# Transposes of p ahead of a unit's first tile, banks that change places in odd units, and the product by q first on VectorE

## The reference

```python
# 1: a linear attention with complex decays; B, H, S, D = 4, 8, 768, 48
mag = np.sqrt(a_re * a_re + a_im * a_im)
scale = np.minimum(mag, 0.999) / (mag + 1e-06)
for t in range(S):
    new_re = ar * S_re - ai * S_im          # a * scale, at t
    new_im = ar * S_im + ai * S_re
    S_re, S_im = new_re + kv, new_im        # kv: outer product of k and v at t
    y[:, :, t] = np.einsum('bhd,bhde->bhe', q[:, :, t], S_re)
# 2: a feed-forward layer, 384 -> 2048 -> 384, on N = 3072 tokens
h = x @ w_in
g = np.where(h >= 1, h, np.where(h <= -1, 0.0, (h + 1) ** 2 / 4.0))
x = g @ w_out
# 3: eight experts, 384 -> 1024 -> 384, weighted by a normalized gate
P = np.exp(x @ w_gate - max);  8 times: rows, then columns of P normalized
out = sum over e of P[:, e:e + 1] * (np.maximum(x @ w1[e], 0.0) @ w2[e])
```

## Time and profile before

| | |
|---|---|
| median of 3 runs | 2386.37 us (2386.13 to 2387.14) |
| the profiled execution | 2386.86 us, span 2385.1 us |
| TensorE, matmuls | 2261.7 us, 95% of the span |
| VectorE | 1559.6 us, 65% |
| ScalarE | 981.6 us, 41% |
| GpSimd | 461.0 us, 19% |
| mean granted TensorE clock | 0.989 of 2.4 GHz |

### The profile page before, as it was taken

How to read it: one execution, slowest core, us unless ns; L and a number is a source line. 1 busy time by engine, 2 the same in 40 slices (tenths; PEclk the granted TensorE clock), 3 DMA queues, 4 the chain that set the end, 5 groups by cost and what they waited for, 6 DMA issues and landing times.

```text
span 2385.1 us, 43991 instructions
## 1 busy us (share of the span) xinstructions
PE 2261.7 (95%) x16891; PEld 2241.0 (94%) x16891; DVE 1559.6 (65%) x2953; ACT 981.6 (41%) x1675; POOL 461.0 (19%) x325
## 2 busy tenths in 40 slices
PE   2689999999999989999999999999999999999999
PEld 2689999999999889999999999999999999999999
DVE  6898888888874685555556666555556655565553
ACT  2455555555555433333333433333333333333331
POOL 0000000000000312222222222122222222222221
PEclk9799999999999999999999999999999999999999
DMA  3211111111112310011112211110013211111101
GB/s 105 84 33 48 49 49 49 49 50 49 50 37 71 120 54 24 31 54 54 55 54 93 94 54 54 55 53 25 32 54 117 70 54 54 54 54 54 54 1 27
DMA packets 73194, 132.46 MB, mean 56 GB/s; under 512 B 5608, under 2 KB 36584, under 8 KB 72936
## 3 DMA queue, kind: packets, MB, share of 16 engines
q1 hardware_dynamic: 72936, 129.14, 16.4%
HBM read 114.96 MB, written 14.16 MB: 54 GB/s over the span
## 4 chain that ended last, share of the span: by engine, by line
PE 81%; DVE 10%; ACT 7%; issue 2%; DMA 0%; DVEq 0%; ACTq 0%; SPq 0%
PE bank L1431 13%; PE bank L1433 13%; PE bank L1432 13%; PE bank L1598 11%; PE bank L1599 11%; PE bank L1600 11%; PE bank L1412 2%; PE bank L1418 2%; PE bank L1417 2%; PE bank L1422 1%; ACT ubuf L648 1%; ACT ubuf L650 1%; PE bank L1407 1%; ACT ubuf L646 1%; DVE tmp L861 1%
## 5 line engine op out<-in xcount | busy, mean ns | idle before, releaser
L1431 PE MATMUL bank<-x_h,w_h 128*128 128x256 f32 x2112 | 595.8, 282 | 9.0 <-issue 4.1
L1433 PE MATMUL bank<-x_h,w_l 128*128 128x256 f32 x2112 | 595.0, 282 | 0.0
L1432 PE MATMUL bank<-x_l,w_h 128*128 128x256 f32 x2112 | 594.1, 281 | 0.0
L1598 PE MATMUL bank<-w_h,h_h 128*128 128x384 f32 x1536 | 518.2, 337 | 0.4 <-DVE acc L1233 0.4
L1600 PE MATMUL bank<-w_h,h_l 128*128 128x384 f32 x1536 | 515.0, 335 | 0.0
L1599 PE MATMUL bank<-w_l,h_h 128*128 128x384 f32 x1536 | 514.9, 335 | 0.0
L567 POOL TENSOR_TENSOR h_l<-u_s,h_h 128x512 fp32r<-128x512 f32 x192 | 244.6, 1295 | 1136.6 <-ACT h_h L778 1136.6
L1431 PEld LDWEIGHTS bank<-x_h,w_h 128*128 128x128 f32 x2112 | 400.7, 190 | 11.9 <-issue 6.0
L1432 PEld LDWEIGHTS bank<-x_l,w_h 128*128 128x128 f32 x2112 | 401.9, 190 | 0.0
L1433 PEld LDWEIGHTS bank<-x_h,w_l 128*128 128x128 f32 x2112 | 401.5, 190 | 0.0
L1240 DVE SCALAR_TENSOR_TENSOR acc<-bank,prob,acc 128x384 f32<-128x384 f32 x168 | 103.5, 616 | 370.6 <-PE bank L1600 370.6
(11 more groups left out here) (164 smaller groups left out, 4035.8 us busy)
## 6 DMA issues: line engine op xcount, KB each, us to landing
stage<-w_ SPq DMA_DIRECT2D x48, 768.0 KB, 7.9
w_raw<-w_ SPq DMA_DIRECT2D x96, 384.0 KB, 4.8
qb<-q_in_ SPq DMA_DIRECT2D x24, 192.0 KB
kb<-k_in_ SPq DMA_DIRECT2D x24, 192.0 KB
vb<-v_in_ SPq DMA_DIRECT2D x24, 192.0 KB
x_hi<-x2h_s SPq DMA_DIRECT2D x36, 128.0 KB, 1.8
x_lo<-x2l_s SPq DMA_DIRECT2D x36, 128.0 KB, 1.8
x_h<-x_hi SPq DMA_DIRECT2D x6, 768.0 KB, 4.4
```

The costliest lines, as they stand in the source:

```text
L1431: pe.matmul(dst, w[0], x[0], start=first, stop=False)
L1432: pe.matmul(dst, w[0], x[1], start=False, stop=False)
L1433: return pe.matmul(dst, w[1], x[0], start=False, stop=last)
L1598: pe.matmul(dst, h_h[:, f, t_], w2s[slot][0][:, f], start=n == 0, stop=False)
```

## The change

On TensorE steps 0 and 1 stand before the first mm_in of a unit instead of behind it. They wait for p and for state_add of the unit before; for the rest of the unit before step 2 waits. So that this can be, step_bank(u, i) uses the three banks in the order 0, 1, 2 in even units and 0, 2, 1 in odd ones, and step 12 uses the bank of step 10. The gate's matmuls move between steps 0 and 1, ahead of mm_in, and write into columns that step 1 leaves alone.

On VectorE the product by q is the first of the unit, ahead of gate_out and g_lo(t-1). p_inv of an even unit moves from the end of the odd unit before into the even unit, behind g_lo(t-1). final moves ahead of state_add at an odd unit's end. scale(u + 3) moves ahead of g_max(t+3) and x_lo.

On ScalarE, in even units: p_sq behind g_hi(t), stacks(u, 1) ahead of p_root, scale_sq(u + 3) ahead of g_sq(t+2), scale_root(u + 3) ahead of g_hi(t+2).

```diff
+        def step_bank(u, i):
+            return att[(i if u % 2 == 0 else -i) % 3] if i < 12 else step_bank(u, 10)
...
@@ ScalarE, unit(u) @@
                 stacks(u, 0)
-                if even:
+                if even and not moe:
                     p_sq(u + 1)
...
                 if u > 2:
                     g_hi(t)
+                if even and moe:
+                    p_sq(u + 1)
                 if moe:
                     g_sq(t + 1)
+                stacks(u, 1)
                 if even:
                     p_root(u + 1)
-                stacks(u, 1)
                 if moe:
                     g_hi(t + 1)
-                    g_sq(t + 2)
                 if even and u + 3 < UNITS:
                     scale_sq(u + 3)
+                if moe:
+                    g_sq(t + 2)
...
+                if even and u + 3 < UNITS:
+                    scale_root(u + 3)
                 if moe:
                     g_hi(t + 2)
                     g_sq(t + 3)
-                if even and u + 3 < UNITS:
-                    scale_root(u + 3)
...
@@ VectorE, unit(u) @@
+                by_qk(u, 0)
+                if not even and u >= 5:
+                    gate_out(u // 2 - 2)
+                if u == 1:
+                    scale(3)
                 if u > 2:
                     g_lo(t - 1)
-                if not even and u >= 5:
-                    gate_out(u // 2 - 2)
-                by_qk(u, 0)
-                if u == 1:
-                    scale(3)
+                if even:
+                    p_inv(u)
                 if u > 2:
                     g_max(t)
...
                 if scans:
                     scan(pair, 1, 4)
+                    final(u + 1)
                 state_add(u)
...
-                if scans:
-                    final(u + 1)
+                if even and u + 3 < UNITS:
+                    scale(u + 3)
                 if moe:
                     g_max(t + 3)
...
                 x_lo(u)
-                if even and u + 3 < UNITS:
-                    scale(u + 3)
-                if scans:
-                    if u + 3 < UNITS:
-                        scale_sum(u + 3)
-                    p_inv(u + 1)
+                if scans and u + 3 < UNITS:
+                    scale_sum(u + 3)
...
@@ TensorE @@
                 if i == 0:
                     pe.wait_ge(p_done, u + 1)
-                    if u:
-                        pe.wait_ge(dve_ev, d)
-                        pe.wait_ge(act_ev, a)
-
+                if i == 1 and u:
+                    pe.wait_ge(dve_ev, (u - 1) * DVE_EV + 7)
+                    if u % 2 and u >= 5:
+                        gate(u // 2 - 2)
                 if i == 2:
+                    pe.wait_ge(act_ev, a)
                     pe.wait_ge(dve_ev, d + 2)
...
-            STEPS_AT = [(), (0, 1), (2, 3), (4, 5), (6, 7), (8, 9), (10, 11), (12,)]
+            STEPS_AT = [(0, 1), (), (2, 3), (4, 5), (6, 7), (8, 9), (10, 11), (12,)]
```

More of the change, by code:

```diff
@@ L627, in stacks @@
                     act.activation((qs, ks)[half][0:96, 4 * n:4 * n + 4],
-                                   att[i % 3][0:96, :].rearrange("p (h t) -> p h t", h=4), ACT.Copy)\
+                                   step_bank(u, i)[0:96, :].rearrange("p (h t) -> p h t", h=4), ACT.Copy)\
                        .then_inc(act_ev, 1)
@@ L632, in y_out @@
                 act.wait_ge(step_done, u * STEPS + (12 if u < 2 else 11))
-                act.activation(y, att[1][:, 0:DM], ACT.Copy).then_inc(act_ev, 1)
+                act.activation(y, step_bank(u, 10)[:, 0:DM], ACT.Copy).then_inc(act_ev, 1)
             def x_hi(u):
@@ L637, in x_hi @@
                 act.activation(xh[:, u // 2 % 2, :, of_unit(u, 128)],
-                               att[0][:, 0:DM].rearrange("p (k t) -> p k t", k=KT), ACT.Copy).then_inc(act_ev, 1)
+                               step_bank(u, 12)[:, 0:DM].rearrange("p (k t) -> p k t", k=KT), ACT.Copy)\
+                   .then_inc(act_ev, 1)
             def g_sq(t):
@@ L961, in bound @@
                 dve.wait_ge(step_done, u * STEPS + 6)
-                dve.tensor_reduce(r_sum[0:1, u:u + 1], att[2][0:1, DM:DM + KT + 1], AX.X, ALU.add).then_inc(bound_done, 1)
+                dve.tensor_reduce(r_sum[0:1, u:u + 1], step_bank(u, 5)[0:1, DM:DM + KT + 1], AX.X, ALU.add)\
+                   .then_inc(bound_done, 1)
             def by_qk(u, half):
@@ L978, in masked @@
                     dve.wait_ge(step_done, u * STEPS + 9 + n)
-                    dve.tensor_tensor(at[:, 4 * n:4 * n + 4], att[(8 + n) % 3][:].rearrange("p (h t) -> p h t", h=4),
-                                      mask[:].unsqueeze(1).to_broadcast([128, 4, 128]), ALU.mult).then_inc(dve_ev, 1)
+                    dve.tensor_tensor(at[:, 4 * n:4 * n + 4],
+                                      step_bank(u, 8 + n)[:].rearrange("p (h t) -> p h t", h=4), mask[:].unsqueeze(1).to_broadcast([128, 4, 128]), ALU.mult).then_inc(dve_ev, 1)
             def state_add(u):
@@ L984, in state_add @@
                 dve.wait_ge(step_done, u * STEPS + 12)
-                dve.tensor_tensor(state[0:96, b, 0:DM], att[2][0:96, 0:DM], state[0:96, b, 0:DM], ALU.add).then_inc(dve_ev, 1)
+                dve.tensor_tensor(state[0:96, b, 0:DM], step_bank(u, 11)[0:96, 0:DM], state[0:96, b, 0:DM], ALU.add)\
+                   .then_inc(dve_ev, 1)
             def x_lo(u):
@@ L1362, in att_step @@
                 d, a = u * DVE_EV, u * ACT_EV
-                dst = att[i % 3]
+                dst = step_bank(u, i)
                 if i == 0:
                     pe.wait_ge(p_done, u + 1)
-                    if u:
-                        pe.wait_ge(dve_ev, d)
-                        pe.wait_ge(act_ev, a)
+                if i == 1 and u:
+                    pe.wait_ge(dve_ev, (u - 1) * DVE_EV + 7)
+                    if u % 2 and u >= 5:
+                        gate(u // 2 - 2)
                 if i == 2:
+                    pe.wait_ge(act_ev, a)
                     pe.wait_ge(dve_ev, d + 2)
+                if i == 4:
+                    pe.wait_ge(pinv_done, u + 1)
                     if u % 2 and u >= 5:
                         pe.wait_ge(lg_done, u // 2 - 1)
-                if i == 4:
-                    pe.wait_ge(pinv_done, u + 1)
                 if i == 5:
@@ L1470, in gate @@
                     tok = slice(b * 128, (b + 1) * 128)
-                    o = b * 2 * E
+                    o = DM + b * 2 * E
                     for n in range(KT):
@@ L1489, in _ @@
                         mm_in(t)
-                    if s == 0 and u % 2 and u >= 5:
-                        pe.wait_ge(dve_ev, (u - 1) * DVE_EV + 7)
-                        gate(u // 2 - 2)
                     for i in STEPS_AT[2 * s + 1]:
```

6 lines of the change are left out of this document (3 added, 3 removed).

## The result

The changed kernel takes 2406.64 us (median of four runs, 2402.94 to 2407.74), the kernel before, run beside it, 2386.25 us (four runs, 2384.96 to 2387.14). The ratio is 1.0083, with an interval from 1.0066 to 1.0101: the change makes the kernel 20 us slower. The forecast was 2412 us.

A forecast was written before the change was run, and what follows sets the result against it. TensorE, busy 95% of the span, was taken to bound the kernel, so its work and gaps count. 2386.9 + 15 (waits in nine pairs) + 10 (clock) + 0 (other units) = 2412 us; 8 in 10 range 2391 to 2425.

The forecast's parts named there:

- What the change removes: TensorE's gaps per pair of units: on qt 1.31 and 0.95, on ks 0.95; together 3.2 us removed.
- Step 1, pinv: Even unit: p_inv behind the product by q and g_lo makes TensorE wait 0.8 us for pinv (0 to 1.5).
- Step 2, kt: Even unit: final's first instruction, held beside GpSimd's pinv, delays the product by k; new TensorE wait 1.35 us.
- Step 3, at: Even unit: masked ends at 291.17, TensorE would be there at 291.06; new wait 0.1 us (0 to 0.9).
- Step 4, x2l_s: Even unit: squaring waits for the decays' reload, g_sq through x2_lo queue behind; first mm_out waits 2.6 us (0.9 to 3.5).
- Step 5, the odd unit: Odd unit: product by q comes without a gap, kt and at just in time; 0.05 us added; pair 61.0.
- The other units: Units 1, 2, 22 and 23, outside the nine full pairs: together 0 us, from -4 to +2.
- The clock: TensorE's clock halves for 3.4 us after the 2.6 us gap in two of three pairs, 1.7 us each: +10 us.
- Slower, but at full clock: Rival, chance 0.31: the waits as forecast but no clock drop; 2402 us, from 2393 to 2407.
- Faster: Rival, chance 0.13: reload no obstacle, x2_lo done by 298.5, 2.6 us sooner; 2378 us, at best 2352.
- It evens out: Rival, chance 0.06: hold shorter than in unit 2 (-1.05) and x2_lo 1 us earlier; 2387 us.
- worse: Rival, chance 0.05: the odd unit's thin margins go too, by a us each; over 2425 us.

The follow-up runs named there:

- steps_back: Changed kernel with squaring behind third g_sq, p_inv ahead of g_lo, and TensorE's steps 0 and 1 behind mm_in again: 2360.3 us; in five rounds 2359.0.
- old_banks: Kernel before, its banks and TensorE order kept, with the change's ScalarE and VectorE order except squaring behind g_sq, p_inv ahead of g_lo: 2363.17 us.
- pinv_first: Changed kernel with p_inv of even units moved ahead of g_lo(t - 1) on VectorE: 2399.64 us, ratio 1.0052.
- x2_first: Changed kernel with scale_sum(u + 3) of even units moved behind x2_lo on VectorE: 2399.76 us, ratio 1.0055.
- sq_back: Changed kernel with scale_sq(u + 3) put back behind g_sq(t + 2) on ScalarE: 2373.23 us, ratio 0.9940.
- two_bufs: Changed kernel with a second buffer for the decays of odd units from unit 5 on, loaded one release earlier: 2374.26 us, ratio 0.9953.
- sq_ahead: Kernel before with only scale_sq(u + 3) moved ahead of g_sq(t + 2) in even units: 2395.89 us, ratio 1.0038.
- ks_first: Kernel before with only stacks(u, 1) moved ahead of p_root on ScalarE: 2381.06 us, ratio 0.9979.
- order_only: Kernel before with stacks(u, 1) ahead of p_root, VectorE's product by q first and even units' p_inv ahead of g_lo: 2382.17 us, ratio 0.9988.

## Why the prediction was right

**What the change removes.** Right: neither qt nor ks is waited for in the steady part, 3.2 us per pair. But the text put the qt gaps down to the early transposes and the order on VectorE together. steps_back and old_banks show that in the steady part the order does it alone.

**Step 1, pinv.** 0.8 forecast, 0.80 in unit 8 (0.74 to 0.91 in nine units). pinv_first removed it by the edit that the step implies.

**Step 2, kt.** 1.35 forecast, 1.31 measured. The hold of final's first instruction by pinv was 1.06 us (1.61 against 0.55), forecast 1.05 from the row of unit 2. A row from another place of the program, of the same two instructions, was a good price. The Trainium skill, "SBUF — State Buffer", section "SBUF: two separate sides", says that a VectorE instruction with two inputs in SBUF and a GpSimd instruction that reads SBUF share a port pair as an exclusive lock, which the one that starts first holds for its whole length. The traces agree: 1.61, 2.20 and 2.19 us beside pinv, and 0.75 in x2_first, where scale_sum came 0.3 us before pinv's end. There state_add and x2_lo, which read one input from a bank, stand beside the same pinv (299.22, 1.83 us) and aren't held:

```profile
299.25 0.55 DVE L994 TENSOR_TENSOR state<-bank,state 96x384 f32<-96x384 f32 x1
299.72 1.07 DVE L1015 TENSOR_TENSOR x2l_s<-bank,x2h_s 128x256 fp32r<-128x256 f32 x3
300.71 0.75 DVE L841 SCALAR_TENSOR_TENSOR sqa<-sqa 128x384 f32<-128x384 f32 x1
```

**Step 3, at.** 0.1 forecast, 0.16 to 0.22 measured.

**Step 4, x2l_s.** ScalarE's wait near 5 forecast and 4.87 measured; VectorE's some 4 and 3.92; the mm_out's 2.6 and 2.1 to 2.3, two of 2.72 and 2.83 behind late reloads (mean of the nine 2.3). The chain of single-buffer reload, squares, g_max, p_inv, scale_sum, x2_lo stood as walked. sq_back and two_bufs, which cut it at two different places, gave back 33 and 32 us, and sq_ahead put it into the kernel before for 9. What the sum could not say, and x2_first did, is that the last link is exchangeable: with scale_sum out of the way the pair is 0.1 us shorter, no more, at full clock.

**Step 5, the odd unit.** No gap, as forecast. The pair came out at 60.97 us against 61.0. That it agrees so closely is in part luck: the new gaps add 4.6 us and not 4.9, while the same matmuls are busy 0.2 to 0.5 us longer in a pair, which the sum didn't have. Over nine pairs the waits make 13.7 us against +15. The other units were put at 0 and cost 1.6: 4.0 lost in the first four units, 2.4 gained behind unit 22's pinv.

**The clock, the term that was mis-sized.** The step said two of three pairs at 1.7 us each, +10. It was three of nine, at 1.3 us each: +4. This term is 6 us too high; the waits are 1 too high and the other units 2 too low, which together is the difference between 2412 and 2407. The step failed in "since 2.6 is beyond both rows": the two gaps of the earlier trace rows, 1.96 and 1.88, were followed by a drop, but six gaps of 2.1 to 2.8 were not. The trace of before already had a third row, which the step left out: a gap of 2.24 us at the start of unit 4, longer than the 1.31 that it took for the longest, with the clock at 1.00 behind it:

```profile
154.26 0.85 PE L1402 MATMUL bank<-ident,p 128*128 128x128 f32 x6 [2.24 <-issue]
...
154.20:157.60 3.40, 2.92 (x24) 2.75 (x24) 2.77 (x7) 2.84 (x6) 1.44 (x1) 1.00 0.00 0
```

The 1.7 was half of 3.4 us. In a pair with a drop the matmuls were busy 1.4 to 1.7 us longer and TensorE 0.1 to 0.3 us less idle, so the pair lost 1.3. The rule quoted from the Trainium skill, "TensorE: Matmul & The Clock Gate", Part 1, was read as a drop in all nine pairs; as read there, it fell, since six of nine passed. In pinv_first, where less wait lies ahead of the gap in the unit, there were more drops and not fewer, which speaks against that reading too.

**The rivals.** *Slower, but at full clock* (2402, up to 2407) is as near to the result as the forecast (2412, from 2407): 2406.64 lies on the border of the two, and six of nine pairs are of the rival's kind. The case was put as one thing or the other, and the kernel did both, so the forecast's direction and waits are confirmed, its clock only in part. *Faster* would have needed x2_lo 2.6 us sooner than walked. That is what two_bufs and sq_back do, and they gave 2374 and 2373, where this rival had 2378. *It evens out* and *worse* didn't come.

**What stays open.** Why some gaps of 2.1 us drop the clock and others of 2.83 and 2.96 don't. Why the granted clock of the first units differs from kernel to kernel, which moved ks_first and order_only by some 3 us. And why unit 2 of ks_first starts 2.5 us later than before.

## What to carry to other kernels

Before a call is moved ahead of another on an engine that works in order, look up in the trace what it waits for: here a preparation for three units later, of which nobody was in need, was put ahead of the current tile's squares, and its wait for a buffer's reload went through three engines' queues to TensorE. The wait that the profile names on the busiest engine is where the loss comes to light; removing that one wait may only move it (x2_first), so cut the chain at its head, by order or by a second buffer. Where a change has many parts, take each one back by itself: here two of the three parts in its title, the early transposes and the banks, were worth 2 to 3 us, the reordering of the helper engines, with the product by q as its named part, 24, and two small moves hid all of it by costing 47.

## What the runs showed of the hardware

**The clock lets long gaps pass.** Of the gaps on x2l_s in the steady part, those of 2.06 to 2.96 us were followed by a drop to half in 3 of 9 cases in the changed kernel, in 6 of 9 in pinv_first and in 1 of 2 in sq_ahead; those of 1.40 to 1.63 us in none of 7, and the other gaps from unit 4's pinv to the attention's end, 1.32 us and less, in none. The three longest, 2.72, 2.83 and 2.96, all passed. In the first units the same wait of 1.85 us, for g_l at 151 us, was followed by a drop in steps_back and not in old_banks, and the one before unit 4's transposes of p was let pass at 2.24 us in the kernel before and at 2.01 in ks_first, but not at 1.98 in sq_ahead. A drop lasted 3.4 us in most cases and cost a pair 1.3 us in the changed kernel and 1.5 to 1.6 in pinv_first; one of 10.2 us cost 4.5 (63.9 against 59.36). The gaps of 1.9 us of the earlier trace rows made it look certain. The length of a gap alone doesn't tell.

**A held instruction costs the rest of its blocker's time.** VectorE's instructions beside GpSimd's pinv (1.83 us) took 1.61 and 2.20 instead of 0.55 us, and in the changed kernel both ended 0.4 us after pinv did (283.32 + 1.83 against 283.96 + 1.61, 303.55 + 1.82 against 303.58 + 2.20); this could be taken from one kernel to the next like any other duration. Instructions of VectorE with one input in a bank were not held beside it (0.55 and 1.07 us in x2_first).
